# The weight-value product of an attention loop as two 128x64 tiles of the array, with TensorE's loop written out

## What is computed

```python
scores = scale * np.matmul(q, k.transpose(0, 1, 3, 2))
keep = is_global | is_local          # the first 8 keys, and the 96 up to the query
scores = np.where(keep, scores - slope * dist, -1e9)
a = np.exp(scores - scores.max(-1)); a = a / (a.sum(-1) + 1e-9)
out = np.matmul(a, v)
```

## Time and profile before

| what | value |
|---|---|
| three runs | 607.34, 607.75, 607.88 us; median 607.75 |
| profiled execution, first to last instruction | 608.0 us (the profile states no other time of it) |
| mean granted TensorE clock | 0.994 |
| TensorE matmul busy | 573.1 us (94%) |
| VectorE busy | 295.0 us (49%) |
| ScalarE busy | 163.4 us (27%) |
| attention with its tail | 0 to about 141.5 us |
| feed-forward layer (L596, L608) | 155.2 to 422.7 us |

### The profile page before, as it was taken

The page is one execution under the profiler, slowest core; times in us unless marked ns, Lnnn a source line. Parts: engine busy times, 40 slices in busy tenths (PEclk is TensorE's granted clock), DMA queues, the critical chain, the costliest instruction groups (busy, mean ns, idle before and its releaser), DMA issues.

```text
span 608.0 us, 10353 instructions
## 1 busy us (share of the span) xinstructions
PE 573.1 (94%) x3401; PEld 540.0 (89%) x3401; DVE 295.0 (49%) x729; ACT 163.4 (27%) x377; POOL 281.0 (46%) x289
## 2 busy tenths in 40 slices
PE   2989899999999999999999999999997997997997
PEld 2889888968999999999999999999996995895896
DVE  5878787866422222222222222222376476287175
ACT  2766766725311110101110111110221220211221
POOL 7546555217710034000991056860597696488000
PEclk9999999999999999999999999999999998999999
DMA  5588877244220004000252000000001001000101
GB/s 104 135 177 162 140 140 146 68 140 130 81 69 0 0 1 138 0 0 0 72 185 88 0 0 0 1 0 1 1 1 52 0 0 49 3 1 10 42 0 52
DMA packets 50084, 33.25 MB, mean 55 GB/s; under 512 B 39688, under 2 KB 39696, under 8 KB 50064
## 3 DMA queue, kind: packets, MB, share of 16 engines
q1 hardware_dynamic: 47504, 26.72, 17.2%
q10 hardware_dynamic: 2560, 6.29, 4.6%
HBM read 23.57 MB, written 3.15 MB: 44 GB/s over the span
## 4 chain that ended last, share of the span: by engine, by line
PE 69%; DVE 10%; issue 9%; DMA 6%; ACT 4%; ACTq 1%; DVEq 0%; POOL 0%; SPq 0%; POOLq 0%
PE bank L596 22%; PE bank L608 22%; PE bank L662 6%; DMA q_lh<-q_hl 5%; PE bank L638 4%; PE bank L647 4%; PE bank L479 3%; DVE gate_exp L1084 2%; DVE k_square L1092 2%; ACT HH L819 2%; PE bank L582 2%; PE bank L442 2%; PE bank L501 2%; PE bank L425 1%; PE bank L453 1%
## 5 line engine op out<-in xcount | busy, mean ns | idle before, releaser
L1065 DVE SCALAR_TENSOR_TENSOR HL<-bank,HH 128x384 fp32r<-128x384 f32 x64 | 35.7, 558 | 172.0 <-ACT HH L803 172.0
L803 ACT ACTIVATE HH<-bank 128x384 fp32r<-128x384 f32 x64 | 31.5, 492 | 231.2 <-PE bank L596 231.2
L596 PE MATMUL bank<-UH,w1h 128*128 x256 | 86.3, 337 | 0.0
L608 PE MATMUL bank<-HL,w2h 128*128 128x384 f32 x256 | 86.1, 336 | 0.0
L596 PE MATMUL bank<-UH,w1l 128*128 x256 | 86.0, 336 | 0.0
L596 PE MATMUL bank<-UL,w1h 128*128 x256 | 85.9, 335 | 0.0
L608 PE MATMUL bank<-HH,w2h 128*128 128x384 f32 x256 | 85.8, 335 | 0.0
L608 PE MATMUL bank<-HH,w2l 128*128 128x384 f32 x256 | 85.8, 335 | 0.0
L1203 POOL TENSOR_SCALAR w1h<-raw 128x2048 fp32r<-128x2048 f32 x5 | 9.6, 1914 | 162.9 <-PE bank L608 140.8
L720 ACT ACTIVATE probs<-probs,neg_max 128x256 f32<-128x256 f32 (+1 forms) x96 | 41.9, 485 | 33.9 <-DVE neg_max L886 33.9
L647 PE MATMUL bank<-WVH,HH 128*128 128x512 f32 x96 | 38.5, 401 | 11.5 <-DVE HL L1096 11.5
(11 more groups left out here) (128 smaller groups left out, 1277.5 us busy)
## 6 DMA issues: line engine op xcount, KB each, us to landing
raw<-in_moe_w_ch SPq DMA_DIRECT2D x8, 1024.0 KB, 5.3
q_lh<-q_hl ACTq DMA_DIRECT2D x32, 192.0 KB, 4.3
q_nat<-in_q SPq DMA_DIRECT2D x16, 192.0 KB, 4.6
k_nat<-in_k SPq DMA_DIRECT2D x16, 192.0 KB, 5.4
v_all<-in_v SPq DMA_DIRECT2D x16, 192.0 KB, 3.1
out<-result SPq DMA_DIRECT2D x12, 256.0 KB, 2.0
raw<-in_moe_w_v SPq DMA_DIRECT2D x2, 1024.0 KB, 5.3
raw<-in_moe_w_k SPq DMA_DIRECT2D x2, 1024.0 KB, 5.0
```

The lines of the kernel that those rows point to most:

```text
L596: mm = pe.matmul(bank[4 + f % 2][:, 0:BLK], w[:, kt, f * P:(f + 1) * P], x[:, kt, ds(blk * BLK, BLK)], start=kt == 0 and n == 0, stop=kt = ...
L608: mm = pe.matmul(bank[d][:, 0:BLK], w[:, f, d * P:(d + 1) * P], x[:, f % 2, :], start=f == 0 and n == 0, stop=f == FQ - 1 and n == 2)
L803: act.activation(HH[:, f % 2, :], bank[4 + f % 2][:, 0:BLK], ACT.Relu).then_inc(hid_high, 1)
L1065: dve.scalar_tensor_tensor(out=HL[:, f % 2, :], in0=bank[4 + f % 2][:, 0:BLK], scalar=0.0, in1=HH[:, f % 2, :].bitcast(F32), op0=ALU.max, ...
```

## The change

Each weight-value product of 128 queries becomes two of 64: queries 0 to 63 go to PSUM partitions 0 to 63, queries 64 to 127 to partitions 64 to 127, each with 64 columns of `probs_t` as weights and the same 96 moving columns. These are 128x64 tiles of the array. The transposes and the scores stay 128x128. TensorE's `Fori` over pairs 1 to 6 becomes a Python loop over all pairs, so its waits and addresses are constants; the loops of ScalarE and VectorE stay.

```diff
-                        mm = pe.matmul(bank[6 + n % 2][:, i * WIDE:(i + 1) * WIDE],
-                                       probs_t[:, n % 2, c * P:(c + 1) * P], src, start=c == places[0],
-                                       stop=c == places[-1])
+                        for rows in (slice(0, P // 2), slice(P // 2, P)):
+                            mm = pe.matmul(bank[6 + n % 2][rows, i * WIDE:(i + 1) * WIDE],
+                                           probs_t[:, n % 2, c * P + rows.start:c * P + rows.stop], src,
+                                           start=c == places[0], stop=c == places[-1])
                 mm.then_inc(pv_done, 1)
...
-                pair(0)
-                with pe.Fori(1, PAIRS - 1) as p:
+                for p in range(PAIRS):
                     pair(p)
-                pair(PAIRS - 1)
                 turn(PAIRS - 1, 4)
                 weigh(PAIRS - 1, 3)
```

## The result

| kernel | median, range, executions | ratio to before, 95% interval |
|---|---|---|
| before | 608.87 us (606.66 to 611.66, 13) | |
| after | 614.45 us (610.91 to 616.43, 13) | 1.0066 [1.0040, 1.0093] |

The change makes the kernel slower by 0.7%. The ratio is not the quotient of the two medians, which is 1.0092: the executions of after spread over 5.5 us, and the quotient of the means is 1.0070. The median of before is here 608.87 us, 1.1 above that of the three runs that the prediction had. The profiled execution of after took 615.87 us with a span of 614.1 us, 6.1 more than that of before, at a mean granted clock of 0.989.

What follows compares the result with a forecast made beforehand. Attention was taken as bound in turn by TensorE with VectorE, swap DMAs, then TensorE or VectorE; +0.8, +1.1, +0.7, +0.4 and +0.5 made +3.5 us on 607.75, so 611.2 us, range 605.8 to 622.

Steps and rivals of the forecast that it cites:

- the sum: Attention's added terms: +0.8 first heads, +1.1 swap heads, +0.7 and +0.4 next two, +0.5 last weighs, together +3.5 us.
- The bound: In attention no single engine: order of waits decides; inside a head VectorE never waits for TensorE, only at its start.
- The regimes: Attention heads: three by TensorE and VectorE in turn (20.08 us), seven by swap DMAs (51.61 us), then TensorE, VectorE, TensorE.
- The signs: Right: TensorE heads 7.0 to 7.1 us, VectorE waiting inside heads. Wrong: halves starting together, weigh under 0.88 us, VectorE without waits.
- The product: One weight-value product in a weigh, as four 64-column loads and matmuls: stays 0.22 us, ends -0.06 and +0.10.
- the first rival: Halves' matmuls run side by side without a drain: product 0.16 us, -1.5 us, 606.3 us, faster; chance 0.22.
- The change of shape: Going into and out of 64-column tiles, three times a head: 0.24 us a weigh, ends 0 and 0.56.
- The third step's scores: In swap-bound heads, scores 0.48 us late against a 0.06 margin: +0.42 a round, less 0.1, so +0.32.
- The longer program: TensorE's written-out loop makes more instructions, read in the background: priced at nothing.
- (a): Halves' matmuls side by side and no drain at shape changes: -1.5 us, 606.3 us, faster; chance 0.22.
- (b): Halves stream one after the other, 0.32 us a product: +14.2 us, 622 us, or 614 without shape cost; chance 0.20.
- (c): Overlapping half loads pay for the drain, only the loop's branches are won: -0.8 us, 607.0 us, no change; chance 0.25.

## Why the prediction was right, and where its steps were not

The forecast was 611.2 us and slower with 0.53, within 605.8 to 622.0. It was measured at 614.45 and slower. The number came out right by luck, on a wrong account: the cost that decided was one that the sum had at nothing, and the +3.5 us that it did have can't be seen once that cost is away.

- **The bound.** The regimes held: heads of TensorE at its own length or at that of a swap, VectorE unslowed inside. The swaps' heads took 50.06 us for seven (57.82 to 107.88) where 51.61 had stood; that says nothing of the edit, as the kernel before without TensorE's dense program has 48.32 there.
- **The signs.** Those named for the account being wrong came: the halves' matmuls start together, four products take 0.66 us and not 0.88, and VectorE inside a head waits as before. The heads were to be 7.0 to 7.1 us between 36 and 57 us; two of the three are 6.64.
- **The product.** Taken as 0.22 us, "nothing gained or lost", with -0.06 and +0.10 as ends. It was 0.164, the lower end. The step that failed is "If a load costs by its columns, loads stay at 4 x 0.055": two loads on different columns overlap and a pair takes 0.082. What the Trainium skill, TensorE: Matmul & The Clock Gate, section Part 3: Packing small matmuls, says of tiles side by side stood behind the first rival; the trace agrees, with starts 6 to 7 ns apart.
- **The change of shape.** Taken as 0.24 from one row of eight partitions, measured 0.31 to 0.33, and 0.30 in the kernel with twice the switches. The Trainium skill, TensorEngine Tiling (Array Packing), section Key Properties, has a change of tiling mode drain TensorE; these gaps agree. The two mis-sized terms go against each other: the weighs' 3 x 0.31 us are paid back in part by 11 x 0.058, and TensorE's head was 6.64 where the sum had 7.06.
- **The third step's scores.** Put at 0.48 late, +0.32 a round. By the loads they came 0.21 later in the head (112.43 - 107.88 = 4.55, before 112.77 - 108.43 = 4.34), and VectorE's steps grew by 0.07 at most. The +3.5 us of the sum can't be seen: without the jump, halves and written loop together give 1.0023 to 1.0035, and whole products with the written loop 1.0021.
- **The longer program.** "I price that at nothing", since the straight code of L501 ran evenly and a stall would show as idle TensorE without a releaser. The stall did show in just that way, 2.97 us, but in a place where the row could not speak for it: not in straight code but at a jump. To it belong 1.7 us at 1.2 GHz. By medians the jump costs 4.4 us (614.4 against 610.0), by ratios 0.45% or 2.7 us (mean of 1.0066 and 1.0082 against that of 1.0023 and 1.0035). Six of the 13 executions of after took 610.9 to 612.5 us and the other seven 614.5 to 616.4, as if the gap were not there every time; the nine of its repetition show no such division, and only the two profiled ones can be looked into.
- **The rivals.** None held as written. (a) had the product right (side by side) and no drain, which was wrong. (b) needs serial streams, which the kernel with the halves in the other order has for most of a weigh. (c), loads of the halves paying for the drain, comes nearest: they pay two thirds of it; its 607.0 us missed the jump.

**What stays open.** Why kernels with TensorE's loop written out and no dear jump sit at 1.002 to 1.003, and the one with whole products and its dense program at 1.0046. That the piece of instructions was held up by the weight load: it is read from two traces that agree (136.4 and 138.4 us) and from the start of the kernel, where loads end at about 9 us and pieces come 1.7 to 1.9 us behind the jumps instead of 4.1 to 4.3, but the load was never moved away by itself, and in before and in the kernel with whole products and the written loop the piece came (135.70 and 139.53 us) within the last microsecond of that load, not behind it. That halves would keep their worth under the hardware loop was not tried: their partitions come from constants in this kernel.

## What to carry to other kernels

Whoever writes a loop out should look at the end of the branch that holds it. A jump over code that never runs can land in instructions that are no longer at hand; here it cost 2.7 to 4.4 us, at a moment when large loads filled the DMA engines. Leaving the unused code out cured it, and so did putting the program that runs last, so that it falls through; but do the latter only on engines that have slack at the start, for on VectorE the same edit cost more than it could bring. Halving a matmul's output side pays only where neighbours in the program use different columns of the array, and where a run of them is long enough to pay 0.30 to 0.33 us for the way in and out (here 0.058 a product: about six products break even, and a weigh has three or four).

## What the runs showed of the hardware

- A jump over unexecuted code took 0.31 us (before), 0.73 (whole products, loop written), 6.41 and 6.64 (after) on TensorE, and VectorE stood still for 3.84 us behind its own at the start. TensorE works again 2.5 us after a 16 KB piece begins to arrive (136.48 to 138.97, 138.40 to 140.92), VectorE 2.2 us after an 8 KB piece (8.85 to 11.02).
- Behind the idle stretch TensorE was granted 1.2 GHz for 3.4 us in both traces of after; the stretch of six matmuls before it had run at 2.4.
- Float32 tiles of 128x64 on different columns start 6 to 7 ns apart and a pair takes 0.082 us for 96 columns in both; on the same columns each one takes 0.082 us for itself. With all low halves of a weigh before all high ones, the high stream began while three of the eight low matmuls were still to start, so a product took 0.25 us and not 0.33.
- Changing from full matmuls to such tiles costs 0.20 us, and back about 0.13.
